# Attention of 48 heads: another order of the instructions on four engines, and a third buffer for raw q and k

## The chip, the cores and the metric

The kernel runs on one core of a Trainium2 chip. The metric is the device time of one execution in microseconds, the median of the runs. A core has five engines that run side by side, each through its own list of instructions in a fixed order: TensorE (PE in the profile, PEld its weight loads), VectorE (DVE), ScalarE (ACT), GpSimd (POOL) and SyncE (SP, which here only issues DMAs). They wait for one another by semaphores. SBUF is the memory on the core, PSUM the one into which TensorE writes.

## The reference, cut to what matters

```python
batch, n_heads, seq, head_dim = (4, 12, 448, 64)
...
def rmsnorm(x, g):
    rms = np.sqrt(np.mean(x * x, axis=-1, keepdims=True) + 1e-06)
    return x / rms * g
q_n, k_n = (rmsnorm(q, g_q), rmsnorm(k, g_k))
scale = 1.0 / np.sqrt(q.shape[-1])
scores = scale * np.matmul(q_n, k_n.transpose(0, 1, 3, 2))
scores = scores - np.max(scores, axis=-1, keepdims=True)
attn = np.exp(scores)
attn = attn / (np.sum(attn, axis=-1, keepdims=True) + 1e-09)
return np.matmul(attn, v).astype(np.float32)
```

Behind the attention follow a mixture of eight experts with one expert for each token (1792 tokens of width 768) and a feed-forward layer (768 to 2048 to 768). The change does not touch these two.

## The kernel before, in words

`attention` works through N = 48 heads of 448 rows and 64 columns. A head's rows lie on 112 partitions, four on each (T = 4, R = 112), so a head has four quarters t = 0 to 3 of 112 rows. All five engines run a loop over m, one round for a head, but at different depth: in round m the scores and the softmax are those of head m, preparation belongs to heads m + 1 to m + 3, values and outputs to head m - 1 and m - 2. What stands in a round, and in which order, is written out by hand for each engine; this order is what the engine does.

One head n passes through these steps:

- `load` (SP): q and k into `qk_raw`, then v into `v_raw`. SP's queue goes on with `store` of an older head and, in fourteen rounds, with a chunk of the experts' weights (`w_raw`, L118). Before it loads q and k of head n, SP waits until GpSimd has normalised q and k of head n - 2, and before v until GpSimd has split v of head n - 2.
- `square` (ACT), `fold_squares` (POOL), `sum_squares` (DVE, sumsq), `invert_rms` (POOL, meansq and rstd): the factors of the norm.
- `norm_k` and `norm_q` (POOL): k_nn (k twice side by side) and q_n.
- `transpose_k` and `transpose_q` (PE) into the PSUM tile `ps_tr`, which both use in turn. `copy_k` (ACT, kT_hi) and `split_k` (DVE, kT_lo) split k in a high and a low part, `copy_q` (ACT, qT_hi) and `split_q` (DVE, qT_lo) q.
- `scores` (PE) in two calls, g = 0 for quarters 0 and 1, g = 1 for quarters 2 and 3; "first" and "second scores" below.
- `row_max` (DVE, neg_max), `exp` (ACT, probs) for each quarter.
- `transpose_p` (PE) for each quarter into one of two PSUM banks of `ps_pt`; `split_hi` (ACT, pT_hi) and `split_lo` (DVE, pT_lo) take them out. Quarter t may be transposed once quarter t - 2 has been taken out.
- `split_v` (ACT, then POOL, v_hl), `values` (PE) in two halves of four matmuls, `copy_u` (ACT, u_sb), `outputs` (PE), `guard_sums` (POOL), `invert_sums` and `store_x` (DVE, x_tok).

Buffers with a number are used in turn by even and odd heads, among them `qk_raw0` and `qk_raw1`.

Of the kernel before, what the change touches and what calls it, by code (L numbers as in the profile page):

```python
# [14 lines left out]
def attention(nc, consts, q, k, v, g_q, g_k, emb, tau, w1, w2, x_tok, x_rows, w1_raw, w2_raw, s_first, s_x_out):  # L15
# [3 lines left out]
    N = B * H  # L19
# [11 lines left out]
    with ExitStack() as ctx:  # L31
# [5 lines left out]

        qk_raw = [sb(f"qk_raw{u}", [R, 2, T, D]) for u in range(2)]
        v_raw = [sb(f"v_raw{u}", [R, T, D]) for u in range(2)]
# [39 lines left out]
        s_gain_in, s_gain = sem("s_gain_in"), sem("s_gain")  # L79
        s_qk_in = [sem(f"s_qk_in{u}") for u in range(2)]  # L80
        s_v_in = [sem(f"s_v_in{u}") for u in range(2)]
# [11 lines left out]
        def _(sp):  # L93
            def load(n, u):

                if n > 1:
                    sp.wait_ge(s_qn, n - 1)
                    sp.wait_ge(s_kn, n - 1)
                for i, src in enumerate((qd, kd)):
                    sp.dma_start(qk_raw[u][:, i, :, :], src[bass.ds(n, 1), :, :, :].rearrange("o p t d -> p (o t) d")).then_inc(s_qk_in[u], 16)  # L100
                if n > 1:
                    sp.wait_ge(s_vhl, n - 1)
                sp.dma_start(v_raw[u][:, :, :], vd[bass.ds(n, 1), :, :, :].rearrange("o p t d -> p (o t) d")).then_inc(s_v_in[u], 16)
# [37 lines left out]
        def _(pool):  # L141
# [38 lines left out]
            def norm_k(n, u):  # L180
                pool.wait_ge(s_r, n + 1)
                if n > 1:
                    pool.wait_ge(s_trk, n - 1)
                for a in range(2):
                    last = pool.tensor_tensor(k_nn[u][:, :, a, :], qk_raw[u][:, 1, :, :], factors(u, 1), ALU.mult)
                last.then_inc(s_kn, 1)

            def norm_q(n, u):
                if n > 1:
                    pool.wait_ge(s_trq, n - 1)  # L190
                pool.tensor_tensor(q_n[u][:, :, :], qk_raw[u][:, 0, :, :], factors(u, 0), ALU.mult).then_inc(s_qn, 1)

            pool.wait_ge(s_half, 3)
            for m in range(-2, N):
# [4 lines left out]
                if m + 2 < N:  # L199
                    invert_rms(m + 2, (m + 2) % 2)  # L200
                if 0 <= m + 1 < N:
                    split_v(m + 1, (m + 1) % 2)
                if m + 2 < N:
                    norm_k(m + 2, (m + 2) % 2)
                if m >= 0:
# [5 lines left out]
        def _(pe):  # L211
# [67 lines left out]

            for m in range(-1, N + 1):  # L280
                if 0 <= m < N:
                    scores(m, m % 2, 1)
                if m + 1 < N:
                    transpose_k(m + 1, (m + 1) % 2)
                if 0 <= m < N:
                    transpose_p(m, m % 2, 0)
                if m - 1 >= 0:
                    values(m - 1, (m - 1) % 2, 0)
                    values(m - 1, (m - 1) % 2, 1)
                if m + 1 < N:  # L290
                    transpose_q(m + 1, (m + 1) % 2)
                if 0 <= m < N:
                    transpose_p(m, m % 2, 1)
                    transpose_p(m, m % 2, 2)
                if m + 1 < N:
                    scores(m + 1, (m + 1) % 2, 0)
                if 0 <= m < N:
                    transpose_emb(m, m % 2)
                    transpose_p(m, m % 2, 3)
# [4 lines left out]
        def _(act):  # L304
            def square(n, u):
                act.wait_ge(s_qk_in[u], fills(n, u, 32))
                if n > 1:
                    act.wait_ge(s_fold, n - 1)
                flat = qk_raw[u][:, :, :, :].rearrange("p a t d -> p (a t) d")
                act.square(squares[u][:, :, :], flat).then_inc(s_sq, 1)  # L310
# [52 lines left out]
            for m in range(-2, N + 2):  # L363
# [7 lines left out]
                if 0 <= m < N:  # L371
                    exp(m, m % 2, 0)
                    exp(m, m % 2, 1)
                if 0 <= m + 1 < N:
                    copy_k(m + 1, (m + 1) % 2)
                if 0 <= m < N:
                    exp(m, m % 2, 2)
                    split_hi(m, m % 2, 0)
                if 0 <= m + 1 < N:
                    copy_q(m + 1, (m + 1) % 2)  # L380
                    split_v(m + 1, (m + 1) % 2)
                if 0 <= m < N:
                    split_hi(m, m % 2, 1)
                if m + 3 < N:
                    square(m + 3, (m + 3) % 2)
                    square_emb(m + 3, (m + 3) % 2)

        @block.vector
        def _(dve):
# [72 lines left out]
            for m in range(-2, N + 2):  # L462
                if 0 <= m - 1 < N:
                    split_lo(m - 1, (m - 1) % 2, 2)
                    split_lo(m - 1, (m - 1) % 2, 3)
                if m - 2 >= 0:
                    store_x(m - 2, (m - 2) % 2)
                if 0 <= m < N:
                    row_max(m, m % 2, 2)
                if m + 2 < N:  # L470
                    sum_squares(m + 2, (m + 2) % 2)
                    prepare(m + 2, (m + 2) % 2)
                if 0 <= m - 1 < N:
                    invert_sums(m - 1, (m - 1) % 2)
                if 0 <= m < N:
                    row_max(m, m % 2, 3)
                if 0 <= m + 1 < N:
                    split_k(m + 1, (m + 1) % 2)
                if 0 <= m < N:
                    split_lo(m, m % 2, 0)  # L480
# [1136 lines left out]
```

## Time and profile before

| | us |
|---|---|
| median of 3 runs (lowest, highest) | 1323.76 (1323.04, 1324.76) |
| profiled execution: own time | 1325.78 |
| profiled execution: span | 1324.1 |
| TensorE busy in the span | 1222.3 (92%) |
| VectorE busy | 903.3 (68%) |
| ScalarE busy | 751.2 (57%) |
| GpSimd busy | 525.6 (40%) |
| attention, first to last x_tok and its stores | about 0 to 382 |

The span runs from the first to the last instruction; the execution's own time holds some 2 us around it. Busy time is an average over stages with different limits. A line of the timeline gives the start and the duration of an instruction, its engine, its line in the kernel, what it writes and reads, how many such instructions are merged in the line (x4), and in brackets how long the engine stood idle before it and which instruction released it. A duration reaches to the acknowledged write, so the next instruction of an engine often starts before the one ahead has ended; what an instruction costs on its engine is the distance from start to start.

### The profile page before, as it was taken

Reading aid. Unit: us, or ns where it says so; the run is one execution under the profiler, and the core shown is the slowest. Engines: PE = TensorE matmul, PEld = TensorE weight load, DVE = VectorE, ACT = ScalarE, POOL = GpSimd, SP = SyncE. Lnnn points to the kernel's source line nnn. Section 1 sums busy time; section 2 is a strip of 40 time slices with the busy share of each in tenths; the row PEclk is TensorE's granted clock in tenths of the full one; section 3 lists DMA queues with packets and bytes.
Section 4 is the critical chain, followed back from the end, with each engine's and each line's share of the span. In section 5 each row is a group of like instructions: output and inputs, shape, how many; then the busy total and the mean of one; then the engine's idle time right before and its main releaser. Section 6 shows DMA issues by size and latency. Waiting matters only on the chain. (4 is left out here: it accounts for less than half of the span.)

```text
span 1324.1 us, 21194 instructions
## 1 busy us (share of the span) xinstructions
PE 1222.3 (92%) x6986; PEld 1077.5 (81%) x6986; DVE 903.3 (68%) x1305; ACT 751.2 (57%) x1434; POOL 525.6 (40%) x533
## 2 busy tenths in 40 slices
PE   4898989898955999999999995999999999999998
PEld 3777777777744888999889995899999999999997
DVE  5888888888864999999999993455432235552222
ACT  4888888888864777877778874222241122221111
POOL 5767676767613777667676761000000000000000
PEclk8999999999966999999999997999999999999999
DMA  1233333322201455555554114111232222211132
GB/s 49 73 95 98 102 87 88 86 65 61 56 11 36 157 206 188 211 192 187 195 197 176 49 45 134 29 56 49 62 111 59 85 72 69 75 49 46 56 85 71
DMA packets 99979, 126.45 MB, mean 95 GB/s; under 512 B 28568, under 2 KB 81048, under 8 KB 99872
## 3 DMA queue, kind: packets, MB, share of 16 engines
q1 hardware_dynamic: 92416, 103.07, 25.4%
q0 software_dynamic: 3360, 16.52, 3.4%
q10 hardware_dynamic: 4096, 5.51, 1.2%
q8 instruction: 58, 0.95, 0.3%
q14 instruction: 49, 0.40, 0.1%
HBM read 193.88 MB, written 19.27 MB: 161 GB/s over the span
## 5 line engine op out<-in xcount | busy, mean ns | idle before, releaser
L1017 ACT CAST w_hi<-w_raw 128x768 fp32r<-128x768 f32 (+1 forms) x294 | 249.4, 929 | 12.9 <-DMA w_raw<-moe_w_in 11.7
L1087 DVE TENSOR_TENSOR w_lo<-w_raw,w_hi 128x1024 fp32r<-128x1024 f32 x84 | 188.7, 2282 | 9.7 <-POOL w_lo L906 7.0
L1497 DVE TENSOR_TENSOR out_lo<-out_raw,out_hi 128x384 fp32r<-128x384 f32 x64 | 35.7, 558 | 169.5 <-ACT out_hi L1406 169.5
L1288 PE MATMUL ps_acc<-yT_hi,in_hi 128*128 128x448 f32 x384 | 143.0, 372 | 2.1 <-DVE yT_lo L1483 2.1
L1318 PE MATMUL ps_acc<-gT_hi,out_hi 128*128 128x448 f32 x384 | 142.6, 371 | 0.0
L906 POOL TENSOR_TENSOR w_lo<-w_raw,w_hi 128x1024 fp32r<-128x1024 f32 x42 | 104.4, 2487 | 95.1 <-ACT w_hi L1017 95.1
L1289 PE MATMUL ps_acc<-yT_hi,in_lo 128*128 128x448 f32 x384 | 141.9, 370 | 0.0
L1290 PE MATMUL ps_acc<-yT_lo,in_hi 128*128 128x448 f32 x384 | 141.9, 370 | 0.0
L1320 PE MATMUL ps_acc<-gT_lo,out_hi 128*128 128x448 f32 x384 | 140.5, 366 | 0.0
L1319 PE MATMUL ps_acc<-gT_hi,out_lo 128*128 128x448 f32 x384 | 140.4, 366 | 0.0
L1400 ACT ACTIVATE small_h<-ps_acc 128x448 f32<-128x448 f32 x64 | 35.0, 546 | 183.4 <-PE ps_acc L1290 183.4
L1406 ACT CAST out_hi<-out_raw 128x384 fp32r<-128x384 f32 x64 | 32.9, 513 | 179.9 <-PE ps_acc L1320 179.6
L1096 DVE TENSOR_TENSOR w_lo<-w_raw,w_hi 128x768 fp32r<-128x768 f32 x126 | 133.3, 1122 | 0.0
L407 DVE TENSOR_TENSOR pT_lo<-ps_pt,pT_hi 112x448 fp32r<-112x448 f32 x192 | 115.5, 622 | 22.3 <-ACT pT_hi L354 16.0
L345 ACT ACTIVATE probs<-ps_s,neg_max 112x448 f32<-112x448 f32 x192 | 123.4, 657 | 3.5 <-DVE neg_max L401 3.5
L401 DVE TENSOR_REDUCE neg_max<-ps_s 112x1 f32<-112x448 f32 x192 | 113.6, 613 | 9.3 <-PE ps_s L222 4.5
L246 PE MATMUL ps_pt<-ident,probs 112*112 112x112 f32 x768 | 101.3, 265 | 20.0 <-ACT probs L345 19.2
L1505 DVE TENSOR_TENSOR g_sb<-ps_acc,small_h 128x448 f32<-128x448 f32 x64 | 40.0, 625 | 116.2 <-ACT small_h L1400 116.2
L990 PE MATMUL ps_y<-w_hi,hT_hi 128*128 128x384 f32 x336 | 116.8, 348 | 1.5 <-issue 1.3
L900 POOL TENSOR_TENSOR w_lo<-w_raw,w_hi 128x768 fp32r<-128x768 f32 x42 | 106.8, 2544 | 19.0 <-ACT w_hi L1017 17.3
L991 PE MATMUL ps_y<-w_lo,hT_hi 128*128 128x384 f32 x336 | 113.5, 338 | 0.0
L992 PE MATMUL ps_y<-w_hi,hT_lo 128*128 128x384 f32 x336 | 113.5, 338 | 0.0
(184 smaller groups left out, 2903.8 us busy)
## 6 DMA issues: line engine op xcount, KB each, us to landing
w_raw<-moe_w_in SPq DMA_DIRECT2D x84, 1536.0 KB
in_raw<-moe_w_in_in SPq DMA_DIRECT2D x32, 384.0 KB, 3.3
out_raw<-moe_w_out_in SPq DMA_DIRECT2D x64, 192.0 KB, 2.4
qk_raw<-q_in SPq DMA_DIRECT2D x48, 112.0 KB, 2.1
qk_raw<-k_in SPq DMA_DIRECT2D x48, 112.0 KB, 2.2
v_raw<-v_in SPq DMA_DIRECT2D x48, 112.0 KB, 2.0
x_rows<-x_tok SPq DMA_DIRECT2D x48, 112.0 KB, 2.5
out_rows<-o_sb ACTq DMA_DIRECT2D x26, 168.0 KB, 2.4
```

The lines of the kernel that those rows point to most:

```text
L345: act.activation(probs[:, t, :], ps_s[0:R, t, 0:S], ACT.Exp, bias=neg_max[u][:, t:t + 1], accum_out=sums[u][:, t:t + 1]).then_inc(s_exp, 1)
L407: dve.tensor_tensor(pT_lo[u][:, :, cols], src, pT_hi[u][:, :, cols].bitcast(F32), ALU.subtract).then_inc(s_plo, 1)
L990: pe.matmul(out, hT_hi[u][:, c, :], w2_hi[:, c, cols], start=c == 0, stop=False)
L1017: act.copy(out[:, c, :], raw[:, c, :]).then_inc(s_hi, 1)
L1087: dve.tensor_tensor(w1_lo[:, c, :], w1_raw[:, c, :], w1_hi[:, c, :].bitcast(F32), ALU.subtract).then_inc(s_w1lo, 1)
L1096: dve.tensor_tensor(w2_lo[:, c, :], w2_raw[:, c, :], w2_hi[:, c, :].bitcast(F32), ALU.subtract).then_inc(s_w2lo, 1)
L1288: pe.matmul(h, in_hi[u][:, c, :], yT_hi[:, c, cols], start=c == 0, stop=False)
L1289: pe.matmul(h, in_lo[u][:, c, :], yT_hi[:, c, cols], start=False, stop=False)
L1290: last = pe.matmul(h, in_hi[u][:, c, :], yT_lo[:, c, cols], start=False, stop=c == C - 1)
L1318: pe.matmul(acc, out_hi[u][:, lhs], hi, start=first, stop=False)
L1319: pe.matmul(acc, out_lo[u][:, lhs], hi, start=False, stop=False)
L1320: last = pe.matmul(acc, out_hi[u][:, lhs], lo, start=False, stop=final)
```

## The change

Nothing is added to the computation or taken from it. Five things move and one buffer is added:

- TensorE: k of head m + 2 is transposed directly behind the first scores of head m + 1, half a round earlier than before; q's transposes stand between the two halves of the values.
- ScalarE: the second exponential moves behind k's copy; the squares stand directly behind q's copy, ahead of v's and of the pT_hi of quarter 1.
- VectorE: sumsq stands ahead of x_tok, and kT_lo directly behind x_tok, both ahead of the max of quarter 2.
- GpSimd: norm_k stands ahead of split_v.
- `qk_raw` has three buffers, and SP waits for the norms of head n - 3.

```diff
-        qk_raw = [sb(f"qk_raw{u}", [R, 2, T, D]) for u in range(2)]
+        qk_raw = [sb(f"qk_raw{w}", [R, 2, T, D]) for w in range(3)]
...
-                if n > 1:
-                    sp.wait_ge(s_qn, n - 1)
-                    sp.wait_ge(s_kn, n - 1)
+                if n > 2:
+                    sp.wait_ge(s_qn, n - 2)
+                    sp.wait_ge(s_kn, n - 2)
...
+                if m + 2 < N:
+                    norm_k(m + 2, (m + 2) % 2)
                 if 0 <= m + 1 < N:
                     split_v(m + 1, (m + 1) % 2)
-                if m + 2 < N:
-                    norm_k(m + 2, (m + 2) % 2)
...
-            for m in range(-1, N + 1):
+            for m in range(-2, N + 1):
                 if 0 <= m < N:
                     scores(m, m % 2, 1)
-                if m + 1 < N:
-                    transpose_k(m + 1, (m + 1) % 2)
-                if 0 <= m < N:
                     transpose_p(m, m % 2, 0)
                 if m - 1 >= 0:
                     values(m - 1, (m - 1) % 2, 0)
+                if 0 <= m + 1 < N:
+                    transpose_q(m + 1, (m + 1) % 2)
+                if m - 1 >= 0:
                     values(m - 1, (m - 1) % 2, 1)
-                if m + 1 < N:
-                    transpose_q(m + 1, (m + 1) % 2)
...
-                if m + 1 < N:
+                if 0 <= m + 1 < N:
                     scores(m + 1, (m + 1) % 2, 0)
+                if m + 2 < N:
+                    transpose_k(m + 2, (m + 2) % 2)
...
                     exp(m, m % 2, 0)
-                    exp(m, m % 2, 1)
                 if 0 <= m + 1 < N:
                     copy_k(m + 1, (m + 1) % 2)
                 if 0 <= m < N:
+                    exp(m, m % 2, 1)
                     exp(m, m % 2, 2)
...
                     copy_q(m + 1, (m + 1) % 2)
+                if m + 3 < N:
+                    square(m + 3, (m + 3) % 2)
+                    square_emb(m + 3, (m + 3) % 2)
+                if 0 <= m + 1 < N:
                     split_v(m + 1, (m + 1) % 2)
                 if 0 <= m < N:
                     split_hi(m, m % 2, 1)
-                if m + 3 < N:
-                    square(m + 3, (m + 3) % 2)
-                    square_emb(m + 3, (m + 3) % 2)
...
-                if m - 2 >= 0:
-                    store_x(m - 2, (m - 2) % 2)
-                if 0 <= m < N:
-                    row_max(m, m % 2, 2)
                 if m + 2 < N:
                     sum_squares(m + 2, (m + 2) % 2)
                     prepare(m + 2, (m + 2) % 2)
+                if m - 2 >= 0:
+                    store_x(m - 2, (m - 2) % 2)
+                if 0 <= m + 1 < N:
+                    split_k(m + 1, (m + 1) % 2)
+                if 0 <= m < N:
+                    row_max(m, m % 2, 2)
                 if 0 <= m - 1 < N:
                     invert_sums(m - 1, (m - 1) % 2)
                 if 0 <= m < N:
                     row_max(m, m % 2, 3)
-                if 0 <= m + 1 < N:
-                    split_k(m + 1, (m + 1) % 2)
-                if 0 <= m < N:
                     split_lo(m, m % 2, 0)
```

VectorE in the middle of the attention, before the change, from the maxima of quarters 0 and 1 of a head to its pT_lo of quarter 0 (the number behind a tile's name is the buffer, even or odd head):

```order
L401 TENSOR_REDUCE neg_max0<-ps_s 112x1 x2
L407 TENSOR_TENSOR pT_lo1<-ps_pt,pT_hi1 112x4x112 x2
L425 TENSOR_TENSOR x_tok<-ps_ux,inv_sums0 112x4x72
L401 TENSOR_REDUCE neg_max0<-ps_s 112x1
L394 TENSOR_REDUCE sumsq0<-folded0 112x8
L420 RECIPROCAL inv_sums1<-sums_eps1 112x4
L401 TENSOR_REDUCE neg_max0<-ps_s 112x1
L411 TENSOR_TENSOR kT_lo1<-ps_tr,kT_hi1 128x448
L407 TENSOR_TENSOR pT_lo0<-ps_pt,pT_hi0 112x4x112
```

The same stretch after the change:

```order
L402 TENSOR_REDUCE neg_max0<-ps_s 112x1 x2
L408 TENSOR_TENSOR pT_lo1<-ps_pt,pT_hi1 112x4x112 x2
L395 TENSOR_REDUCE sumsq0<-folded0 112x8
L426 TENSOR_TENSOR x_tok<-ps_ux,inv_sums0 112x4x72
L412 TENSOR_TENSOR kT_lo1<-ps_tr,kT_hi1 128x448
L402 TENSOR_REDUCE neg_max0<-ps_s 112x1
L421 RECIPROCAL inv_sums1<-sums_eps1 112x4
L402 TENSOR_REDUCE neg_max0<-ps_s 112x1
L408 TENSOR_TENSOR pT_lo0<-ps_pt,pT_hi0 112x4x112
```

sumsq has moved ahead of x_tok and kT_lo ahead of the first of the two single maxima, which is that of quarter 2; the one behind the reciprocal is that of quarter 3.

ScalarE, before, from q's copy of one head to the exponential of quarter 3:

```order
L354 CAST pT_hi0<-ps_pt 112x4x112
L336 ACTIVATE qT_hi1<-ps_tr,gain 128x224
L322 CAST v_hl1<-v_raw1 112x4x64
L354 CAST pT_hi0<-ps_pt 112x4x112
L310 ACTIVATE squares1<-qk_raw1 112x512
L345 ACTIVATE probs,sums0<-ps_s,neg_max0 112x448
```

And after the change:

```order
L345 ACTIVATE probs,sums0<-ps_s,neg_max0 112x448 x2
L354 CAST pT_hi0<-ps_pt 112x4x112
L336 ACTIVATE qT_hi1<-ps_tr,gain 128x224
L310 ACTIVATE squares1<-qk_raw1 112x512
L322 CAST v_hl1<-v_raw1 112x4x64
L354 CAST pT_hi0<-ps_pt 112x4x112
L345 ACTIVATE probs,sums0<-ps_s,neg_max0 112x448
```

The squares have moved two places forward. At the top, two exponentials now stand behind k's copy: those of quarters 1 and 2.

TensorE, before, from the two p transposes of quarters 1 and 2 (x8) over a whole half round to k's transposes:

```order
L246 MATMUL ps_pt<-ident,probs 112x112 x8
L222 MATMUL ps_s<-kT_hi0,qT_hi0 112x448 x2
L222 MATMUL ps_s<-kT_lo0,qT_hi0 112x448 x2
L222 MATMUL ps_s<-kT_hi0,qT_lo0 112x448 x2
L246 MATMUL ps_pt<-ident,probs 112x112 x4
L268 MATMUL ps_ux<-mix,u_sb 112x72 x4
L222 MATMUL ps_s<-kT_hi0,qT_hi0 112x448 x2
L222 MATMUL ps_s<-kT_lo0,qT_hi0 112x448 x2
L222 MATMUL ps_s<-kT_hi0,qT_lo0 112x448 x2
L230 MATMUL ps_tr<-ident,k_nn1 128x112 x4
L246 MATMUL ps_pt<-ident,probs 112x112 x4
```

And after the change, from the same place:

```order
L246 MATMUL ps_pt<-ident,probs 112x112 x8
L222 MATMUL ps_s<-kT_hi0,qT_hi0 112x448 x2
L222 MATMUL ps_s<-kT_lo0,qT_hi0 112x448 x2
L222 MATMUL ps_s<-kT_hi0,qT_lo0 112x448 x2
L230 MATMUL ps_tr<-ident,k_nn1 128x112 x4
L246 MATMUL ps_pt<-ident,probs 112x112 x4
L268 MATMUL ps_ux<-mix,u_sb 112x72 x4
L222 MATMUL ps_s<-kT_hi0,qT_hi0 112x448 x2
L222 MATMUL ps_s<-kT_lo0,qT_hi0 112x448 x2
L222 MATMUL ps_s<-kT_hi0,qT_lo0 112x448 x2
L246 MATMUL ps_pt<-ident,probs 112x112 x4
```

k's transposes have moved from behind the second scores (the rows that follow u_sb's) to behind the first.

## Rows read from the trace of the kernel before

**Rows 1.** Windows: length; busy (count) of PE, PEld, DVE, ACT, POOL; clock; DMA; GB/s.

```profile
200.00:250.00 50.00, 44.61 (x339) 36.43 (x336) 42.88 (x88) 43.74 (x116) 35.54 (x56) 1.00 0.32 88
```

**Rows 2.** Timeline, TensorE: start, duration, instruction, count, idle before and its releaser.

```profile
99.84 0.46 PE L222 MATMUL ps_s<-kT_hi,qT_hi 64*112 64x448 f32 x2 [0.32 <-DVE qT_lo L415]
...
211.82 0.59 PE L246 MATMUL ps_pt<-ident,probs 112*112 112x112 f32 x4 [0.44 <-ACT probs L345]
...
216.65 0.93 PE L246 MATMUL ps_pt<-ident,probs 112*112 112x112 f32 x8
...
217.93 0.46 PE L222 MATMUL ps_s<-kT_hi,qT_hi 64*112 64x448 f32 x2 [0.35 <-DVE qT_lo L415]
...
219.22 0.60 PE L246 MATMUL ps_pt<-ident,probs 112*112 112x112 f32 x4 [0.43 <-ACT probs L345]
```

**Rows 3.** Timeline, ScalarE, one head.

```profile
215.05 0.64 ACT L345 ACTIVATE probs<-ps_s,neg_max 112x448 f32<-112x448 f32 x1
...
215.67 0.54 ACT L354 CAST pT_hi<-ps_pt 112x448 fp32r<-112x448 f32 x1
...
216.85 0.45 ACT L336 ACTIVATE qT_hi<-ps_tr,gain 128x224 fp32r<-128x224 f32 x1 [0.64 <-PE ps_tr L238]
...
217.49 0.53 ACT L354 CAST pT_hi<-ps_pt 112x448 fp32r<-112x448 f32 x1
...
217.91 0.64 ACT L310 ACTIVATE squares<-qk_raw 112x512 f32<-112x512 f32 x1
...
218.45 0.63 ACT L345 ACTIVATE probs<-ps_s,neg_max 112x448 f32<-112x448 f32 x1
```

**Rows 4.** Timeline, VectorE, the same head, then two rows of a late head.

```profile
213.73 0.45 DVE L425 TENSOR_TENSOR x_tok<-ps_ux,inv_sums 112x288 f32<-112x288 f32 x1
...
214.09 0.62 DVE L401 TENSOR_REDUCE neg_max<-ps_s 112x1 f32<-112x448 f32 x1
...
214.63 0.41 DVE L394 TENSOR_REDUCE sumsq<-folded 112x8 f32<-112x256 f32 x1
...
214.96 0.17 DVE L420 RECIPROCAL inv_sums<-sums_eps 112x4 f32<-112x4 f32 x1
...
215.56 0.61 DVE L411 TENSOR_TENSOR kT_lo<-ps_tr,kT_hi 128x448 fp32r<-128x448 f32 x1
...
218.06 0.63 DVE L407 TENSOR_TENSOR pT_lo<-ps_pt,pT_hi 112x448 fp32r<-112x448 f32 x1 [0.27 <-ACT pT_hi L354]
...
218.83 1.16 DVE L401 TENSOR_REDUCE neg_max<-ps_s 112x1 f32<-112x448 f32 x2
...
359.06 1.16 DVE L401 TENSOR_REDUCE neg_max<-ps_s 112x1 f32<-112x448 f32 x2
...
361.19 0.45 DVE L425 TENSOR_TENSOR x_tok<-ps_ux,inv_sums 112x288 f32<-112x288 f32 x1
```

**Rows 5.** Timeline, the last head: a max and the exponential that waits for it.

```profile
368.46 0.61 DVE L401 TENSOR_REDUCE neg_max<-ps_s 112x1 f32<-112x448 f32 x1
...
369.11 0.64 ACT L345 ACTIVATE probs<-ps_s,neg_max 112x448 f32<-112x448 f32 x1 [0.77 <-DVE neg_max L401]
```

**Rows 6.** Timeline, GpSimd, one head.

```profile
217.67 0.73 POOL L148 TENSOR_TENSOR v_hl<-v_raw,v_hl 112x256 fp32r<-112x256 f32 x1 [0.61 <-ACT v_hl L322]
...
218.36 1.18 POOL L185 TENSOR_TENSOR k_nn<-qk_raw,rstd 112x256 f32<-112x256 f32 x2
```

**Rows 7.** Timeline, SP's queue: a weight chunk, and k's load behind it.

```profile
219.38 0.80 SPq L118 DMA_DIRECT2D w_raw<-moe_w_in  x1
...
221.33 0.43 SPq L100 DMA_DIRECT2D qk_raw<-k_in  x1
```

**Rows 8.** Line L100, window 220.9:222: landing of q and k behind this chunk.

```profile
DMA to landing us min/median/max: 2.6/2.7/2.8
```

**Rows 9.** Line L100, window 88:88.9: landing of k behind another chunk, the longest.

```profile
DMA to landing us min/median/max: 2.9/3.5/4.0
```

**Rows 10.** The page's DMA issues: tensors, count, size, median us to landing.

```profile
qk_raw<-k_in SPq DMA_DIRECT2D x48, 112.0 KB, 2.2
```

## What the change does to the time, predicted

> **What bounds the kernel now.** The change touches only the attention stage, the first 380 us of the span, so I read the stage by windows first. In a 50 us stretch from its middle [rows 1] TensorE is busy for 44.6 us, VectorE for 42.9, ScalarE for 43.7, GpSimd for 35.5, at full granted clock. None is full, so the time of a head is set by a loop of waits through several engines. The period comes from the start of the first scores of a head: 99.84 and 217.93, sixteen heads apart, is 7.38 us a head [rows 2].
>
> Next I read the order of time for one head. TensorE transposes the last probabilities at 211.82, works without a gap through outputs, second scores, k's transposes, the next p transpose, eight value matmuls and q's transposes, and starts the next p transposes at 216.65 [rows 2]. ScalarE has stood idle for 0.64 us until q's transposes were done, and copies qT_hi at 216.85; it goes on without a gap through v_hl, pT_hi and squares to the exponential of quarter 3 at 218.45 [rows 3]. That one releases TensorE at 219.22, which waited 0.43 us for it [rows 2]. The loop is 4.83 + 0.20 + 1.60 + 0.77 = 7.40 us, this head's period. VectorE is not in it.
>
> **What the change does to this loop.** Between the two p transposes at 211.82 and 216.65 lie 4.83 us. k's four transposes and half of the eight value matmuls leave this stretch; by their share of it, an estimate, 0.4 and 0.8 us. The k transposes stand where TensorE waited 0.43 us. The squares only swap places with v_hl and pT_hi on ScalarE: the sum to the exponential stays 1.60 us. So this loop falls to about 7.40 - 0.4 - 0.8 = 6.2 us and no longer decides. No operation is added or removed; the price of every edit is one of position.
>
> **What is late next.** The order of VectorE decides. Before, the max of quarter 2 came right behind x_tok, at 214.09; now sumsq, x_tok and kT_lo all stand ahead of it. The exponential of quarter 2 on ScalarE waits for this max, and behind it there are queued pT_hi of quarter 0, qT_hi, squares, v_hl and pT_hi of quarter 1. VectorE then needs the last of these for pT_lo of quarter 1, before it may take the next head's maxima. That is a loop of its own. I add it up from start to start, beginning at the max of quarter 2:
> to its exponential 0.65, as where ScalarE waits for exactly that at 369.11 [rows 5]; exponential to pT_hi 0.62 and pT_hi to qT_hi 0.42 [rows 3]; qT_hi with v_hl 0.64 and squares 0.54, to pT_hi of quarter 1, 1.18 [rows 3]; from there to pT_lo 0.57 (217.49 to 218.06); pT_lo 0.53; the two maxima and two pT_lo that follow, 2.13 (359.06 to 361.19) [rows 4]; sumsq 0.33 and x_tok 0.36 [rows 4]; kT_lo 0.53 (it lasts 0.61 us, as pT_lo does).
> Sum: 0.65 + 0.62 + 0.42 + 1.18 + 0.57 + 0.53 + 2.13 + 0.33 + 0.36 + 0.53 = **7.32 us**.
> A side path is as long. pT_lo of quarter 0 ends at 0.65 + 0.62 + 0.57 + 0.62 = 2.46; p's transpose of quarter 2, which needs its PSUM bank, follows about 0.15 later and takes some 0.4 (two such blocks last 0.93 [rows 2]); scores at about 3.0; the first max 0.90 behind (217.93 to 218.83) at 3.9, against 3.97 on the main path. So 7.32 can be a few hundredths more; less it can be only by the errors of the intervals. Bounds: 7.27 to 7.38. Over the 43 heads in steady state: 0.06 x 43 = **2.6 us gained**, bounds 4.7 and 0.
>
> **The cover of the other moved steps.** k_nn now has to be ready when the first scores have been issued, some 0.8 us after their start; before, the second scores lay between. It ended at 219.54, 1.6 after them, with v_hl's 0.70 and a wait of 0.61 in front [rows 6]. Both are now behind it, and sumsq, which starts the chain, comes 0.9 earlier against the scores. It ends some 0.6 before the scores: 1.4 us of margin, cost nothing; without this cover each 0.1 of lateness would be 0.1 a head. GpSimd's v_hl is then not needed for a head more. q_n and kT_lo are ready before the middle of the values.
>
> **The loads.** On the queue of SP the order stays: v (waits for GpSimd's v_hl), store, in fourteen heads a weight chunk, then q and k, which no longer wait for q_n. The squares are done 0.72 us earlier after qT_hi (0.34 instead of 1.06). And v_hl comes 0.54 later, so v's load and all behind it too. The chunk was issued 2.53 after qT_hi (219.38), is now at 3.07; the squares that need k follow at 7.32 + 0.34 = 7.66, that is 4.59 after the chunk. Without a chunk k is issued near 3.4 and lands 2.2 later, the median [rows 10]: 2 us of margin. With a chunk, k was issued 1.95 behind it and landed at 1.95 + 2.8 = 4.75 after it [rows 7, 8]; the longest of the fourteen is 1.95 + 4.0 = 5.95 [rows 9], the mean over all 5.07. If k stays behind the chunk to the same moment, the squares wait 0.48 on average, 6.7 us in all, on the loop that now decides. If k could land sooner by the whole 0.95 us that it is issued sooner, only the longest would be late, by 0.4. k's 2.8 us against 2.2 without a chunk say that most of its time is the usual latency, and a smaller part queueing; but queueing grows when it is issued sooner. I take a third of the 0.95 as gained: waits of 0 to 1.0, **2.9 us lost**, bounds 0.4 and 6.7.
> The Trainium skill, page DMA: Bandwidth & Descriptors, section Queues, rings and completion order, says that each DMA engine consumes the descriptors of one issuing queue in ring order. By that rule k's bytes stay behind the chunk's however early they are issued, which is the upper bound, and the time would be that of rival 3. The trace agrees in direction: behind the chunk k took 2.8 us instead of 2.2; how it lands when issued sooner, no row shows.
>
> **Start and end.** At the start k's transposes of head 1 stand ahead of the second scores and sumsq and kT_lo ahead of the max, but TensorE waits there anyway: 0, bounds 0.7 either way. In the last heads sumsq (0.33, twice) and kT_lo (0.53) fall away on the new loop, the squares (0.54) mostly on the old one: **0.5 gained**, bounds 0 and 1.2.
>
> **The sum.** -2.6 + 2.9 - 0.5 = -0.2 us. The profiled execution took 1325.8 us with a span of 1324.1; the median of the runs is 1323.8, 2 us less, so I carry the difference over to the median: **1323.6 us**.
>
> **The rivals.**
> 1. The change works as a whole and TensorE's own work becomes the bound. It is busy 44.61 of 50 us [rows 1], 6.58 of 7.38 a head: 0.80 x 43 = 34 us less, 1289. For it: the old loop really shrinks by more than that. Against: the max of quarter 2 is behind three instructions in VectorE's fixed order, and every interval of that loop is measured. 0.10.
> 2. The new loop is as summed, and k lands in time or the waits are absorbed: -2.6 - 0.5, 1320.7. For it: the third buffer lets q and k start right behind the chunk. 0.20.
> 3. The squares wait for k in the chunk heads for the whole time: -2.6 - 0.5 + 6.7 = +3.6, 1327.4. It decides for slower than before once the fourteen waits sum to over 5.7 us, 0.4 each. For it: squares earlier by 0.72, loads later by 0.54, both toward each other. 0.22.
> Left over: the forecast 0.43, and 0.05 for something between the first and the second.
>
> **How the numbers follow.** A measurement of this kernel tells about 0.2% (2.6 us) from no change. The forecast itself spans 1320.5 to 1326.5. Faster holds rival 1, what lies between, and most of rival 2, whose time is just past that line: 0.32. Slower holds most of rival 3 and a little of the forecast: 0.25. No difference: 0.43. Rival 1 is left outside the range; with the loop's bounds added to the rivals 2 and 3 it is 1317 to 1330.
>
> **What the profile after would show.** Right: a period of 7.30 to 7.38; ScalarE idle about 1 us a head ahead of the exponential of quarter 2, released by neg_max; its wait at qT_hi gone; TensorE's wait for the exponential gone, and one before the third p transpose, released by pT_lo, in its place; in chunk heads ScalarE waits ahead of squares for k's load, 0.2 us on average. Wrong: a period under 7.2 and no wait for neg_max (rival 1), no DMA wait at squares (rival 2), or one of 0.5 (rival 3). A GpSimd wait showing at k's transposes would mean that I misjudged its margin.

## The result, and the profile after

| | before | after |
|---|---|---|
| median of 6 runs each, run in turn on one chip | 1324.22 us (1323.04 to 1324.80) | 1330.15 us (1328.41 to 1332.88) |
| ratio, 95% interval | | 1.0048 (1.0034 to 1.0061) |
| profiled execution: own time, span | 1325.78, 1324.1 us | 1328.66, 1326.9 us |

The change makes the kernel slower by 0.5%, some 6 us. I forecast 1323.6 and a range of 1317 to 1330: the range does not hold the time, and the sign is that of rival 3, which I gave 0.22.

The first view is again the windows of the middle stretch. The columns are those of [rows 1].

```profile
200.00:250.00 50.00, 46.28 (x341) 35.54 (x340) 41.03 (x87) 44.19 (x117) 35.18 (x55) 1.00 0.34 89
```

TensorE's granted clock is 1.00 in this stretch of both kernels, and over 40 to 370 us too, so the clock is not the cause. The starts of the first scores give the period. The changed kernel's timeline of TensorE: a wait and the scores behind it, and two starts fourteen heads apart, behind the last long head (the last chunk, issued at 255.76, cost nothing).

```profile
216.83 0.57 PE L246 MATMUL ps_pt<-ident,probs 112*112 112x112 f32 x4 [0.51 <-DVE pT_lo L408]
217.33 0.46 PE L222 MATMUL ps_s<-kT_hi,qT_hi 64*112 64x448 f32 x2
...
254.11 0.46 PE L222 MATMUL ps_s<-kT_hi,qT_hi 64*112 64x448 f32 x2
...
357.14 0.46 PE L222 MATMUL ps_s<-kT_hi,qT_hi 64*112 64x448 f32 x2
```

The last two are 103.03 apart, 7.36 us a head, where [rows 2] gave 7.38. But of the fourteen heads with a chunk nine took longer: 8.23, 8.77, 8.66, 8.26, 8.42, 7.40, 7.94, 7.52 and 7.65. Over 7.36 they sum to 6.6 us. In the wait view of the changed kernel for 0 to 385 us this line names the cause (us in all, number of waits, the longest). Two of its nine waits, 4.8 us and the longest among them, are at the start, as they were before the change, when there were no others; the seven that are new sum to 6.0 us:

```profile
ACT squares L310 <- DMA qk_raw<-k_in: 10.8, 9, 3.4
```

ScalarE's timeline shows one of these waits, and then an undisturbed head to hold against [rows 3]:

```profile
77.70 0.46 ACT L336 ACTIVATE qT_hi<-ps_tr,gain 128x224 fp32r<-128x224 f32 x1
79.51 0.63 ACT L310 ACTIVATE squares<-qk_raw 112x512 f32<-112x512 f32 x1 [1.34 <-DMA qk_raw<-k_in]
...
214.88 0.64 ACT L345 ACTIVATE probs<-ps_s,neg_max 112x448 f32<-112x448 f32 x1 [0.88 <-DVE neg_max L402]
215.50 0.52 ACT L354 CAST pT_hi<-ps_pt 112x448 fp32r<-112x448 f32 x1
215.91 0.46 ACT L336 ACTIVATE qT_hi<-ps_tr,gain 128x224 fp32r<-128x224 f32 x1
216.25 0.64 ACT L310 ACTIVATE squares<-qk_raw 112x512 f32<-112x512 f32 x1
216.77 0.41 ACT L322 CAST v_hl<-v_raw 112x256 fp32r<-112x256 f32 x1
217.07 0.55 ACT L354 CAST pT_hi<-ps_pt 112x448 fp32r<-112x448 f32 x1
```

SP's queue ahead of that wait:

```profile
73.41 0.62 SPq L118 DMA_DIRECT2D w_raw<-moe_w_in  x1
74.13 1.09 SPq L100 DMA_DIRECT2D qk_raw<-q_in  x1
75.26 0.43 SPq L100 DMA_DIRECT2D qk_raw<-k_in  x1
```

And the DMA view of the window 73:80, with the time from issue to landing last:

```profile
w_raw<-moe_w_in SPq DMA_DIRECT2D x1, 512.0 KB, 5.6
...
qk_raw<-k_in SPq DMA_DIRECT2D x1, 112.0 KB, 4.2
```

The chunk is issued at 73.41 and lands 5.6 later, at 79.0. k is issued at 75.26 and lands 4.2 later, at 79.46; the squares start at 79.51. So k landed 6.05 behind the chunk's issue. The squares would have started 0.34 behind qT_hi, as at 215.91 and 216.25, that is at 78.04, 4.63 behind the chunk. I worked out the same distance for all fourteen chunks of both kernels, from SP's timeline and the landing of each single k:

| | k issued behind the chunk's issue | k lands behind the chunk's issue | mean |
|---|---|---|---|
| before, chunks 1 to 5 | 1.82 to 1.99 | 4.93, 5.02, 5.95, 5.19, 5.46 | 5.31 |
| before, chunks 6 to 14 | 1.95 to 2.58 | 4.55 to 5.15 | 4.86 |
| after, chunks 1 to 5 | 1.15 to 2.66 | 5.55, 6.05, 5.98, 5.56, 5.68 | 5.76 |
| after, chunks 6 to 14 | 1.14 to 2.33 | 4.24 to 5.23 | 4.63 |

Over all fourteen the mean is 5.04; before it was 5.02. On average k is issued sooner (1.61 behind the chunk instead of 2.02) and lands no sooner. In all 28 cases k landed behind its chunk, by 0.3 to 1.2 us.

Two things are hidden in these averages. The first six chunks have 512 KB and the other eight 384 KB. By size the means are 5.23 and 4.87 before, 5.60 and 4.62 after; but the sixth, of 512 KB, lands like the small ones (k 4.85 and 4.75 behind it), so size alone does not explain the early ones, and no run separates size from place. And k was not issued much sooner everywhere. In eight heads it was, by 0.7 to 0.8 us. Behind the five chunks of 384 KB among these it landed sooner too, at 4.24 to 4.53, where the same five had 4.55 to 5.05 before; behind the three of 512 KB it did not (5.55, 5.68 and 4.75, before 4.93, 5.46 and 4.85). In the other six heads q's issue took over 1 us, k followed at 1.85 to 2.66 and landed at 4.85 to 6.05.

The page of the changed kernel has the medians (k's stood at 2.2 in [rows 10]):

```profile
qk_raw<-k_in SPq DMA_DIRECT2D x48, 112.0 KB, 2.8
...
w_raw<-moe_w_in SPq DMA_DIRECT2D x6, 512.0 KB, 5.1
```

VectorE in the undisturbed head, to hold against [rows 4]:

```profile
214.23 0.61 DVE L402 TENSOR_REDUCE neg_max<-ps_s 112x1 f32<-112x448 f32 x1
...
216.06 0.62 DVE L408 TENSOR_TENSOR pT_lo<-ps_pt,pT_hi 112x448 fp32r<-112x448 f32 x1 [0.62 <-ACT pT_hi L354]
...
217.65 0.62 DVE L408 TENSOR_TENSOR pT_lo<-ps_pt,pT_hi 112x448 fp32r<-112x448 f32 x1 [0.61 <-ACT pT_hi L354]
218.23 1.16 DVE L402 TENSOR_REDUCE neg_max<-ps_s 112x1 f32<-112x448 f32 x2
219.30 1.15 DVE L408 TENSOR_TENSOR pT_lo<-ps_pt,pT_hi 112x448 fp32r<-112x448 f32 x2
220.36 0.41 DVE L395 TENSOR_REDUCE sumsq<-folded 112x8 f32<-112x256 f32 x1
220.69 0.45 DVE L426 TENSOR_TENSOR x_tok<-ps_ux,inv_sums 112x288 f32<-112x288 f32 x1
221.06 0.62 DVE L412 TENSOR_TENSOR kT_lo<-ps_tr,kT_hi 128x448 fp32r<-128x448 f32 x1
221.59 0.62 DVE L402 TENSOR_REDUCE neg_max<-ps_s 112x1 f32<-112x448 f32 x1
```

From one max of quarter 2 (214.23) to the next (221.59) it is 7.36. The old wait at qT_hi (0.64) is gone; ScalarE waits 0.88 for neg_max, and TensorE waits for pT_lo where it waited for the exponential. The side path adds up to: exponential 0.65, pT_hi 0.62, pT_lo 0.56 and its own 0.62, 0.15 to the p transposes (216.83), 0.50 to the first scores (217.33), 0.90 to the first max (218.23), then 1.07, 1.06, 0.33, 0.37 and 0.53: 7.36, the whole period. On the main path the maxima could have started 0.53 behind 217.65, at 218.18, a few hundredths sooner than they do. With margins this small it takes e1 to tell the two paths apart.

### The profile page after: what moved, and what is told of

It is laid out like the page before. It is cut to its first block and busy times, and to the rows that moved or that the text cites. A ratio compares the mean times of both kernels' runs of the same rounds, so it can differ in the third digit from the quotient of the medians.

```text
span 1326.9 us, 21193 instructions
## 1 busy us (share of the span) xinstructions
PE 1232.0 (93%) x6986; PEld 1072.3 (81%) x6986; DVE 891.8 (67%) x1305; ACT 751.0 (57%) x1434; POOL 529.2 (40%) x533
## 5 line engine op out<-in xcount | busy, mean ns | idle before, releaser
L246 PE MATMUL ps_pt<-ident,probs 112*112 112x112 f32 x768 | 110.3, 267 | 29.5 <-DVE pT_lo L408 29.4
L246 PEld LDWEIGHTS ps_pt<-ident,probs 112*112 112x112 f32 x768 | 79.2, 135 | 60.4 <-issue 33.8
```

The source lines that it names most:

```text
L246: last = pe.transpose(ps_pt[0:R, t % 2, c * R:(c + 1) * R], probs[:, t, c * R:(c + 1) * R], ident[0:R, 0:R])
```

## The experiments

Each was timed in turn with the kernel before. Periods are distances between the starts of the first scores. "Undisturbed" is a head without a wait for a load.

**e1: squares last in ScalarE's round.** Takes them off the main path and 0.8 us further from the load.

```diff
                     copy_q(m + 1, (m + 1) % 2)
-                if m + 3 < N:
-                    square(m + 3, (m + 3) % 2)
...
                     split_hi(m, m % 2, 1)
+                if m + 3 < N:
+                    square(m + 3, (m + 3) % 2)
```

> The changed kernel with one part undone: ScalarE does the squares again last in its round, behind v's copy and pT_hi of quarter 1. Theory A (the loss is ScalarE waiting at the squares for k's load behind a weight chunk, 6.6 us in the trace of the changed kernel): the squares are due 0.7 us later after qT_hi and v's load, the chunk and k are issued 0.5 us earlier, so the wait of 0.2 to 1.3 us in the chunk heads is gone or under 1 us in all. An undisturbed head stays at 7.36 us, because the path over pT_lo of quarter 0, the p transpose of quarter 2, the first scores and the first max (the side path) does not hold the squares. Time about 1330.1 - 6 = 1324, range 1322.5 to 1326. Rival B (the squares' place is harmless; the chunk heads are long because of traffic that SP's queue brings anyway): 1330, no change, and longer chunk heads with another wait. Rival C (the main path of my sum, which holds the squares, decides and not the side path): an undisturbed head also falls by up to 0.5 us, time under 1310.

1324.73 us, 0.9992 (0.9981 to 1.0003) of before. From the fourth head on all take 7.36, and no wait for a load is left. The squares' 0.53 us is gone from the main path and the period has not moved: the side path sets it. VectorE, which in the changed kernel had no wait ahead of the first two maxima, now waits there for the scores:

```profile
220.35 1.16 DVE L401 TENSOR_REDUCE neg_max<-ps_s 112x1 f32<-112x448 f32 x2 [0.47 <-PE ps_s L222]
```

All that the change loses against before sits in the squares' distance to the load.

**e2: the chunk behind q and k in SP's queue.**

```diff
                     .then_inc(s_qk_in[n % 3], 16)
+                if chunk:
+                    chunk()
                 if n > 1:
                     sp.wait_ge(s_vhl, n - 1)
```

> The changed kernel, but SP issues each weight chunk behind the q and k loads of the second head of a pair and ahead of its v load, instead of ahead of the next head's q and k. All else as changed, the squares stay early. Theory A (k late behind the chunk): the waits for k at the squares vanish, undisturbed heads stay at 7.36 us, time 1323 to 1325.5. Now v's load comes behind the chunk, but v has most of a head more to arrive. Rival B (the chunk's bytes themselves, not their place in the queue, disturb): the heads with a chunk stay 0.2 to 1.3 us long, time near 1330. A wait of ScalarE at v's copy would mean that the delay only moved to v.

1324.00 us, 0.9986 (0.9974 to 0.9997). Again 7.36 in all heads from the third on (but the last, 7.08) and no wait for q, k or v. The cause is the place behind the chunk, and either end of the distance mends it. It is the order and not the company: in nine of the fourteen heads the chunk is issued only 0.47 to 0.49 us behind k, and k lands 2.2 to 2.8 us after its issue. With the chunk ahead of it, k took 2.8 to 4.4 us in the changed kernel.

**e3: VectorE takes the max of quarter 2 before kT_lo.** What is late next, by my account, was this max.

```diff
-                if 0 <= m + 1 < N:
-                    split_k(m + 1, (m + 1) % 2)
                 if 0 <= m < N:
                     row_max(m, m % 2, 2)
+                if 0 <= m + 1 < N:
+                    split_k(m + 1, (m + 1) % 2)
```

> The changed kernel, but on VectorE the max of quarter 2 stands ahead of kT_lo instead of behind it (sumsq, x_tok, max, kT_lo). Theory A (the loop that decides runs from the max of quarter 2 over its exponential, pT_hi of quarter 0, pT_lo, p transpose of quarter 2, first scores, the first maxima, two pT_lo, sumsq, x_tok, kT_lo and back to the max): it loses kT_lo's 0.53 us, an undisturbed head falls from 7.36 to about 6.85 us, some 23 us over 44 heads. The chunk waits grow, since k is due 0.5 us sooner: 14 x 0.5 = up to 7 us. Time 1307 to 1316. Rival D (not this order but the work of TensorE, or q's transposes that need kT_lo, decide): the head stays above 7.2 us and TensorE is seen waiting for kT_lo at q's transposes; time 1326 to 1332.

1314.85 us, 0.9911 (0.9891 to 0.9931). Undisturbed heads take 6.93, near the 6.85 expected. But the chunk heads take up to 8.39, one 11.33; the excess over 6.93 sums to some 13 us, where up to 7 was expected.

**e4: max of quarter 2 directly behind x_tok,** ahead of sumsq too (x_tok, max, sumsq, kT_lo).

> The changed kernel with VectorE in the order x_tok, max of quarter 2, sumsq, kT_lo: the order of before, but kT_lo still ahead of the max of quarter 3. Theory A: the loop loses sumsq's 0.33 and kT_lo's 0.53, 7.36 - 0.86 = 6.5; TensorE's own work is 6.6 us a head and sumsq 0.9 later makes k_nn about due, so 6.6 to 6.8 us a head, 26 to 33 us less over 44 heads, and up to 0.7 x 14 = 10 us of chunk waits more. Time 1302 to 1314, and in chunk heads waits of ScalarE for k's load of 1 us and more. Rival D: TensorE waits at q's transposes for kT_lo or at k's transposes for k_nn, and the head stays above 7.1 us; time above 1320.

1330.77 us, 1.0033 (1.0013 to 1.0052): missed. Undisturbed heads take 6.93 as in e3, but the chunk heads take up to 11.31 and four heads behind the last chunk wait for k too; the excess over 6.93 sums to 28 us, where up to 10 was expected. ScalarE's timeline of e4, and the windows around this wait (columns as in [rows 1]):

```profile
60.24 0.63 ACT L310 ACTIVATE squares<-qk_raw 112x512 f32<-112x512 f32 x1 [1.93 <-DMA qk_raw<-k_in]
```

```profile
58.00:60.00 2.00, 2.00 (x18) 1.55 (x16) 0.80 (x2) 0.31 (x1) 1.92 (x3) 1.00 0.47 160
60.00:62.40 2.40, 0.76 (x9) 0.42 (x5) 0.77 (x2) 2.16 (x6) 0.87 (x3) 1.00 0.00 0
62.40:69.50 7.10, 7.10 (x31) 5.96 (x32) 5.43 (x12) 4.82 (x13) 3.84 (x7) 0.53 0.25 65
69.50:75.00 5.50, 5.50 (x46) 4.41 (x45) 4.12 (x10) 4.93 (x14) 2.73 (x5) 0.98 0.44 115
```

Behind the wait of 1.93 us TensorE worked 0.76 of 2.40 us, and then its granted clock was 0.53 on average for 7 us: nearly all at the lower of the two levels, 1.2 instead of 2.4 GHz. This late load cost twice, its wait and the slow matmuls behind it. The 11.33 head of e3 is the same: a wait of 1.93 at its squares, and a granted clock of 0.69 over 206 to 217 us. The changed kernel's waits of up to 1.34 did not do this (clock 1.00 in 79.5 to 86). The length of the wait alone does not decide, though. In e4 the 7 us from the start of the late squares had a clock of 0.69 behind the wait of 1.93, 0.76 behind waits of 1.72, 1.84 and 2.45, but 1.00 behind waits of 1.50, 1.65 and 1.86. The windows behind 1.84 and 1.86:

```profile
127.53:134.53 7.00, 5.43 (x33) 4.27 (x32) 5.32 (x12) 6.11 (x16) 3.27 (x6) 0.76 0.28 66
249.75:256.75 7.00, 5.02 (x38) 4.00 (x37) 5.61 (x13) 6.66 (x18) 3.66 (x6) 1.00 0.27 68
```

**e5: two raw buffers instead of three,** the rest as changed.

> The changed kernel with two raw buffers of q and k instead of three, and SP waiting for the norms of head n - 2 as before the change. The order of all instructions is as in the changed kernel. Theory (k is late because its bytes follow the chunk's, so the moment of its issue matters little): k is issued later by what q waits for q_n, as before the change, 0 to 0.9 us, and lands later by less; excess of the chunk heads 6.6 to 9 us, time 1330 to 1333. Rival (the third buffer lets q be issued directly behind the chunk, where its issue takes 1.1 to 1.6 us, and that delay is the loss): fewer waits with two buffers, 1324 to 1327.

1331.29 us, 1.0047 (1.0034 to 1.0061), the same as the changed kernel; the excess of its heads over 7.36 is 7.1 us, k landed 4.17 to 6.30 behind the chunk. The third buffer is worth nothing here. The rival, that q's early issue is the loss, was not tested by this: q was issued 0.78 to 0.83 us behind the chunk in all but one head (1.25), nearly as early as with three buffers (0.72 to 0.78), and its issue again took up to 1.24 us.

**e6: e2 and e3 together.**

> The changed kernel with two edits together: VectorE's kT_lo behind the max of quarter 2 (as in e3), and the weight chunk issued behind the q and k of its head (as in e2). Theory (the place of the chunk in SP's queue is the only thing that cost e3 time beyond its period of 6.93 us): all heads take 6.93 us, no wait of ScalarE's squares for k, TensorE never at the lower clock in the attention; 44 heads x (7.36 - 6.93) = 19 us below e2's time, that is about 1305. Rival (at 6.93 us a head the loads are late by themselves, because the rounds have become shorter): squares still wait for k in many heads, and the time stays above 1310.

1303.02 us (1302.75 to 1305.67), 0.9841 (0.9827 to 0.9855): as expected, and 22 us under before. From the third head on all but two (7.17 and 7.12) take 6.93, and the last 6.61. The windows of its middle:

```profile
200.00:250.00 50.00, 49.31 (x364) 37.52 (x363) 44.38 (x95) 46.78 (x123) 37.20 (x58) 1.00 0.36 94
```

TensorE is busy for 49.31 of 50 us, against 46.28: what is left to gain in its order is small.

**e7: e2 and e4 together.**

> The changed kernel with VectorE's order x_tok, max of quarter 2, sumsq, kT_lo (as in e4) and the chunk behind q and k (as in e2). Theory: e4's long heads came from the chunk alone, so its undisturbed 6.93 us show in all heads: 1305, the same as the kernel with max before kT_lo and the chunk behind. Rival (sumsq behind the max makes k_nn late, TensorE's k transposes wait for it, as in a third of e4's heads): some 0.1 to 0.2 us a head more, 1309 to 1314.

1308.54 us, 0.9871 (0.9856 to 0.9886), between the two answers. 6.93 in most heads, eight of 7.04 to 8.01. Its wait view has a late k_nn, which the rival named, and waits for k's load:

```profile
PEld ps_tr L233 <- POOL k_nn L188: 26.0, 46, 11.4
...
ACT squares L313 <- DMA qk_raw<-k_in: 8.4, 9, 3.5
```

Both lines hold the start too (11.4 us of the first, 4.8 in two waits of the second). The first line is not the loss: the wait of 0.32 for k_nn stands in heads of 6.93 as well, and in e6 the same weight load (PEld) stands idle for 0.32 with k_nn in time. The long heads are those in which the squares wait for k's load. Waits of 1.10, 0.60, 0.32, 0.74, 0.56, 0.17 and 0.18 go with heads 1.08, 0.58, 0.30, 0.72, 0.55, 0.18 and 0.15 too long. The weight load in a head of 6.93, the longest of these waits and what SP did ahead of that k:

```profile
104.13 0.39 PEld L233 LDWEIGHTS ps_tr<-ident,k_nn 112*128 112x128 f32 x4 [0.32 <-POOL k_nn L188]
```

```profile
110.33 0.63 ACT L313 ACTIVATE squares<-qk_raw 112x512 f32<-112x512 f32 x1 [1.10 <-DMA qk_raw<-k_in]
```

```profile
105.12 1.81 SPq L109 DMA_DIRECT2D x_rows<-x_tok  x1
107.04 0.56 SPq L100 DMA_DIRECT2D qk_raw<-q_in  x1
107.64 0.43 SPq L100 DMA_DIRECT2D qk_raw<-k_in  x1
```

Ahead of the waits of 1.10, 0.60, 0.32 and 0.74 the issue of the store took 1.55 to 1.81 us, ahead of the other three 0.56. So even with e2's order of the queue this kernel still has late loads. The rest of its distance to e6 is the start: its third head begins at 34.03, that of e6 at 31.61.

**e8: e6 and the squares at the end,** as in e1.

> The kernel with max before kT_lo and the chunk behind q and k, and in addition ScalarE's squares at the end of its round, behind the pT_hi of quarter 1 (as in e1). The squares leave the main path (pT_hi of quarter 0, qT_hi, squares, v_hl, pT_hi of quarter 1, pT_lo). If the side path (pT_lo of quarter 0, p's transposes of quarter 2, first scores, first max) sets the 6.93 us, as I read it, the period stays at 6.93 and the time at that of the kernel without this edit, within 2 us. If the main path alone set it, a period of about 6.4, 20 us less.

1317.99 us, 0.9946 (0.9932 to 0.996): both answers missed. The period is 7.25, 0.32 more than with the squares in front. ScalarE's timeline of e8 shows why:

```profile
226.95 0.41 ACT L325 CAST v_hl<-v_raw 112x256 fp32r<-112x256 f32 x1 [0.43 <-PE ps_ux L264]
227.28 0.53 ACT L357 CAST pT_hi<-ps_pt 112x448 fp32r<-112x448 f32 x1
227.71 0.64 ACT L313 ACTIVATE squares<-qk_raw 112x512 f32<-112x512 f32 x1
228.24 0.63 ACT L348 ACTIVATE probs<-ps_s,neg_max 112x448 f32<-112x448 f32 x1
```

v_hl of a head waits until the values of the head two before it have left its buffer. In front of v_hl the squares fill this wait; behind pT_hi they push the exponential of quarter 3. A third loop decides. I read its distances from e8's timelines of ScalarE, VectorE and TensorE, from start to start: pT_hi to the squares 0.43, exponential 0.53, u_sb 0.61, pT_hi 0.41, pT_lo 0.59, sumsq 1.07, x_tok 0.33, max 0.36, kT_lo 0.53, q's transposes 0.76, values 0.15 and 0.69, v_hl 0.45, pT_hi 0.33: 7.24. So the place that the change gives to the squares is right, once the chunk is out of the way.

**e9 to e12: e6 with one part undone.** e9 puts q's transposes back behind both halves of the values, e10 GpSimd's split_v back ahead of norm_k, e11 two raw buffers, e12 kT_lo back behind the max of quarter 3.

```diff
# e9, TensorE
-                if 0 <= m + 1 < N:
-                    transpose_q(m + 1, (m + 1) % 2)
                 if m - 1 >= 0:
                     values(m - 1, (m - 1) % 2, 1)
+                if 0 <= m + 1 < N:
+                    transpose_q(m + 1, (m + 1) % 2)
# e12, VectorE
                     row_max(m, m % 2, 3)
+                if 0 <= m + 1 < N:
+                    split_k(m + 1, (m + 1) % 2)
```

> The best kernel so far (the change, max of quarter 2 before kT_lo, chunk behind q and k: 6.93 us a head, 1303.0 us) with one part of the change undone: TensorE's q transposes behind both halves of the values instead of between them. Theory: q's transposes then start after eight value matmuls, some 1.65 us behind their start, and no longer ScalarE's pT_hi of quarter 0 but they release qT_hi, 0.5 us later than now; squares, v_hl, pT_hi of quarter 1 and pT_lo follow on that path: x_tok to the values 0.51, values 1.65, transposes to qT_hi 0.42, to squares 0.35, v_hl 0.54, pT_hi 0.33, pT_lo 0.56, maxima 0.62, two pT_lo 1.07, sumsq 1.06, x_tok 0.33: 7.44 us a head, about 1326. Rival (ScalarE's slack before v_hl, which waits for the values anyway, takes it up): 6.9 to 7.1, 1303 to 1311.

> The best kernel so far (6.93 us a head, 1303.0 us) with one part of the change undone: GpSimd's v_hl ahead of k_nn, as before the change. Theory: v_hl on GpSimd has to wait for ScalarE's v_hl and takes 0.73 us, so k_nn ends 1.1 us after TensorE could transpose k behind the first scores; TensorE waits there for k_nn every head, second scores and the max of quarter 2 come 0.7 to 1.0 us later: 7.6 to 7.9 us a head, 1333 to 1346. Rival (the wait is absorbed before the second scores, as TensorE idles there anyway): up to 7.1, 1311.

> The best kernel so far (6.93 us a head, 1303.0 us) with two raw buffers of q and k instead of three. Theory: q's load then waits for q_n and is issued 0.8 us later, out of some 1.3 us of margin to the squares: no wait in plain heads, at most a few tenths in chunk heads; 1303 to 1306, the third buffer is not needed. Rival (at the shorter period the margin is gone): squares wait in most heads, 1310 or more.

> The best kernel so far (6.93 us a head, 1303.0 us) with VectorE's kT_lo one place further back, behind the reciprocal and the max of quarter 3, where it stood before the change. Theory: kT_lo starts 0.6 us later, q's transposes (which need the PSUM tile that kT_lo reads) and with them the second half of the values, v_hl and pT_hi of quarter 1 move by 0.5: 7.4 to 7.5 us a head, 1323 to 1328. Rival (only the max of quarter 2 matters and q's transposes have slack): 6.93, 1303.

| | median us | ratio to before, 95% | us a head | expected |
|---|---|---|---|---|
| e9 | 1322.78 | 0.9980 (0.9964 to 0.9995) | 7.35 | 7.44 |
| e10 | 1345.27 | 1.0143 (1.0126 to 1.0159) | 7.83 | 7.6 to 7.9 |
| e11 | 1304.17 | 0.9841 (0.9825 to 0.9858) | 6.93 | 6.93 |
| e12 | 1332.41 | 1.0046 (1.0029 to 1.0062) | 7.53 | 7.4 to 7.5 |

The waits that took over are those named. In e12's timeline of TensorE, q's transposes wait for kT_lo; in e10's wait view for 100 to 330 us, k's wait for k_nn; in e9's, qT_hi waits for q's transposes:

```profile
227.99 0.38 PE L241 MATMUL ps_tr<-ident,q_n 112*128 112x112 f32 x2 [0.67 <-DVE kT_lo L415]
```

```profile
PEld ps_tr L233 <- POOL k_nn L188: 38.9, 29, 1.6
```

```profile
ACT qT_hi L339 <- PE ps_tr L241: 14.8, 32, 0.5
```

e12 is the sharpest: by the ratios to before, one place of kT_lo too far back costs 27 us against e6, one too far forward (e2) 19. The best kernel is e6; e11, with a buffer less, is within their scatter of it.

## Why the prediction was wrong

In the order of its steps. In the profiled runs the last head has its first scores at 371.58 instead of 365.06, 6.5 us later. By the starts of the scores this is: start +0.9, period -1.1 (44 heads of 7.36, before (358.16 - 33.19) / 44 = 7.386), chunk waits +6.6, last head +0.2, within 0.1.

- **The old loop no longer decides: right.** The wait at qT_hi is gone, and e3 and e6 show a period of 6.93 in the same order on TensorE, ScalarE and GpSimd.
- **Late next is the max of quarter 2: right in mechanism, the term mis-sized.** I took 7.32 on the main path and let the side path tie. Measured is 7.36, and the side path decides (e1). I took 0.4 for the p transposes to the scores; it was 0.50. Over the heads that makes 1.1 us gained instead of 2.6, within my bounds of 0 and 4.7.
- **k_nn's cover: right.** No GpSimd wait shows at k's transposes in the steady state; e10 shows what it costs when the cover is gone, 0.90 us a head.
- **The loads: this is the step that failed.** I took "a third of the 0.95 us as gained" and 2.9 us lost. On average neither came: k was issued 0.4 us sooner and not 0.95, because q's issue took over 1 us in six heads, and it landed 5.04 behind the chunk, before 5.02. The waits came to 6.6 us, next to the upper bound of 6.7 that I had set aside. That they meet so closely is partly luck: the bound is fourteen times the mean lateness, which by the measured values is 14 x 0.41 = 5.7, but the five k's that landed ahead of 4.63 gave nothing back. The distance of the squares, 4.59, was right (4.63). My reason was that k's 2.8 us against 2.2 left little for queueing. But that row [rows 8] is of one chunk late in the attention, of 384 KB. The early ones, of 512 KB, of which [rows 9] was one, land k far later: 5.31 behind the chunk on average before, and 5.76 after, where the other nine have 4.86 and 4.63. Against a distance of 4.6 the early five alone cost 5.5 of the 6.6 us. The Trainium skill, page DMA: Bandwidth & Descriptors, section Queues, rings and completion order, says that on each DMA engine the descriptors of a queue are consumed in ring order; the upper bound was what I made of that. The traces agree: in all 28 cases k landed 0.3 to 1.2 us behind the chunk. I had weighed it and gone a third of the way to the other side.
- **Start: 0 taken, 0.9 lost,** a little outside my bound of 0.7: the first scores of the third head are at 34.08 instead of 33.19. The head before them took 9.70 before and 9.98 after, and 8.06 in e6, but 10.67 in e12, where the two heads before it have their first scores at the same times as in e6 (within 0.01). Over all kernels it ran from 8.06 to 11.19, with one profile of each. What decides it stays open.
- **End: 0.5 gained was taken.** The last head itself took 0.2 more (7.08 against 6.90). Behind it the profiled run lost less: the gating's first logits came 4.4 later (386.3 against 381.9), not 6.5. Before, TensorE's granted clock was 0.64 in 372 to 382, with 6.30 us busy; after, it was 0.92 in 378.5 to 388.5, the same place 6.5 us later. The profiled runs as a whole differ by only 2.9 us, the medians by 5.9. The runs of after scatter by 4.5 us, those of before by 1.8; why one profiled run lies below its median I did not test.

With the measured terms, -1.1 + 6.6 + 0.9 and the end at my -0.5, the sum is 5.9 us more, and the medians differ by 5.9. That this agrees to a tenth is luck: the start and the end are from single profiled runs, and these differ by only 2.9 us as a whole. Rival 3 had the mechanism and the price of the waits. Its time, 1327.4, fell short by the two smaller terms, the period and the start. It should have been the forecast: the mean over fourteen landings, 5.07 as I had it, said so already, and nothing but an assumption stood against it.

The gain that the new order allows was hidden by two places: kT_lo one place too early on VectorE, 0.43 us a head, and the chunk one place too early on SP. By the ratios to before, e2 is 0.6% below the changed kernel, e3 1.4% and e6, with both, 2.1%.

## What to carry to other kernels

When a change moves a load's consumer earlier, take the landing as a distance from the large transfer ahead of it in the queue, not from the load's own issue, and look at each instance: the latest ones pay. Put small loads that an engine waits for ahead of a large one of the same queue. When a loop is broken, add up the next one through every instruction that its engines queue ahead of the released one, and try each of these one place to either side: here one place of a 0.5 us instruction was worth 19 and 27 us.

## What the runs showed of the hardware that I had not expected

- SP's issue of q directly behind a chunk lasted 0.31 to 0.95 us before and 0.38 to 1.56 after, when it followed 0.72 instead of 1.6 us behind the chunk's; six of the fourteen took over 1 us. A chunk directly ahead is not needed for it: in the changed kernel k's issue took 1.02 to 1.70 us in nine heads, one of them 30 us behind the last chunk (1.46 at 286.14), and in e2 1.53 at 88.62, nearly 7 us behind one. In e7 such an issue of a store stands ahead of four of the seven late k's. What makes an issue long no run shows.
- Behind a single wait of 1.93 us in ScalarE's stream TensorE's granted clock was 0.53 for 7 us (e4). Behind the changed kernel's waits of up to 1.34 it stayed at 1.00, and so it did in e4 behind one of 1.86, but not behind one of 1.72.
